# Wider spans of keys and fewer groups of queries in a banded attention, with values loaded in smaller pieces

## The reference, cut to what matters

```python
# q, k, v: (2, 8, 768, 64); n_global = 8, n_local = 96
scores = scale * np.matmul(q, k.transpose(0, 1, 3, 2))
rel = pos[:, None] - pos[None, :]
is_global = pos[None, :] < int(n_global)
is_local = (rel >= 0) & (rel < int(n_local))
keep = is_global | is_local
dist = np.where(is_global & ~is_local, float(n_local), np.abs(rel).astype(np.float32))
scores = np.where(keep, scores - slopes * dist, -1e9)
x = softmax(scores) @ v                       # then heads side by side: (2, 768, 512)

u = x + (x^T @ U @ V)^T                       # mixing over the sequence, rank 32
x = u + relu(u @ w_ch1) @ w_ch2               # 512 -> 2048 -> 512

xk = mu_k * x + (1 - mu_k) * x_prev           # x_prev: the row before
xr = mu_r * x + (1 - mu_r) * x_prev
k = relu(xk @ w_k)                            # 512 -> 1024
out = sigmoid(xr @ w_r) * (k * k @ w_v)
```

## Time and profile before

| | us |
|---|---|
| median of 3 runs | 567.49 (566.18 to 567.58) |
| the profiled execution | 570.11 |
| its span | 568.6 |
| granted clock, mean | 0.973 of 2.4 GHz |
| attention, start to about 133 us | 133 |
| matrix products after it | 435 |

### The profile page before, as it was taken

How to read it: one execution, slowest core, us unless ns; L and a number is a source line. 1 busy time by engine, 2 the same in 40 slices (tenths; PEclk the granted TensorE clock), 3 DMA queues, 4 the chain that set the end, 5 groups by cost and what they waited for, 6 DMA issues and landing times.

```text
span 568.6 us, 13272 instructions
## 1 busy us (share of the span) xinstructions
PE 527.8 (93%) x5432; PEld 490.0 (86%) x5432; DVE 192.4 (34%) x527; ACT 139.3 (24%) x408; POOL 248.7 (44%) x251
## 2 busy tenths in 40 slices
PE   2877687798999999999999999999999999999997
PEld 1655566578999999999999999999898898998996
DVE  3547654451222222222212223221253253243122
ACT  2655455551110111111111111112222221321321
POOL 2206812231720090002990056880299599599000
PEclk9879888889999999999999999999999999999999
DMA  8466444510030022000442000000000100101001
GB/s 279 168 251 251 179 178 176 215 56 3 18 131 0 0 75 74 0 0 0 148 148 74 0 1 0 0 0 0 2 1 1 55 0 18 38 1 52 3 0 55
DMA packets 14794, 37.67 MB, mean 66 GB/s; under 512 B 2080, under 2 KB 3360, under 8 KB 13728
## 3 DMA queue, kind: packets, MB, share of 16 engines
q1 hardware_dynamic: 14176, 36.24, 18.0%
q10 hardware_dynamic: 576, 0.84, 0.4%
HBM read 33.92 MB, written 3.15 MB: 65 GB/s over the span
## 4 chain that ended last, share of the span: by engine, by line
PE 92%; issue 4%; DMA 1%; DVE 1%; POOL 0%; ACT 0%; ACTq 0%; DVEq 0%; POOLq 0%
PE psum L525 24%; PE psum L537 23%; PE psum L581 12%; PE psum L590 11%; PE psum L605 6%; PE psum L381 5%; PE psum L393 3%; PE psum L419 2%; DMA k_in<-in_k 1%; PE psum L410 1%; PE psum L436 1%; PE psum L427 1%; PE psum L433 1%; PE psum L434 1%; PE psum L397 1%
## 5 line engine op out<-in xcount | busy, mean ns | idle before, releaser
L929 DVE SCALAR_TENSOR_TENSOR HL<-psum,HH 128x384 fp32r<-128x384 f32 x64 | 35.7, 558 | 176.4 <-ACT HH L724 176.4
L724 ACT ACTIVATE HH<-psum 128x384 fp32r<-128x384 f32 x64 | 31.5, 491 | 235.1 <-PE psum L525 235.1
L525 PE MATMUL psum<-UH,w1h 128*128 (+1 forms) x256 | 86.3, 337 | 1.9 <-POOL UL L1029 1.9
L537 PE MATMUL psum<-HH,w2h 128*128 128x384 f32 x256 | 86.1, 336 | 0.0
L537 PE MATMUL psum<-HL,w2h 128*128 128x384 f32 x256 | 86.1, 336 | 0.0
L525 PE MATMUL psum<-UH,w1l 128*128 (+1 forms) x256 | 86.0, 336 | 0.0
L525 PE MATMUL psum<-UL,w1h 128*128 (+1 forms) x256 | 85.9, 335 | 0.0
L537 PE MATMUL psum<-HH,w2l 128*128 128x384 f32 x256 | 85.8, 335 | 0.0
L1040 POOL TENSOR_SCALAR w1h<-raw 128x2048 fp32r<-128x2048 f32 x5 | 9.6, 1915 | 126.2 <-PE psum L537 126.2
L381 PE MATMUL psum<-k_in,q_in 64*32 64x128 f32 (+1 forms) x1536 | 30.9, 267 | 29.8 <-issue 18.6
L381 PEld LDWEIGHTS psum<-k_in,q_in 64*32 64x32 f32 x1536 | 21.0, 120 | 37.4 <-issue 25.7
(11 more groups left out here) (115 smaller groups left out, 989.5 us busy)
## 6 DMA issues: line engine op xcount, KB each, us to landing
v_in<-in_v SPq DMA_DIRECT2D x8, 1536.0 KB, 6.1
raw<-in_moe_w_ch SPq DMA_DIRECT2D x8, 1024.0 KB, 7.1
out<-result SPq DMA_DIRECT2D x12, 256.0 KB, 2.1
k_in<-in_k SPq DMA_DIRECT2D x7, 432.0 KB, 8.3
q_in<-in_q SPq DMA_DIRECT2D x7, 384.0 KB, 6.9
raw<-in_moe_w_v SPq DMA_DIRECT2D x2, 1024.0 KB, 5.2
raw<-in_moe_w_k SPq DMA_DIRECT2D x2, 1024.0 KB, 5.0
raw<-in_moe_w_r SPq DMA_DIRECT2D x1, 1024.0 KB, 5.1
```

The lines of the kernel that those rows point to most:

```text
L525: mm = pe.matmul(bank[4 + f % 2][:, 0:BLK], w[:, kt, f * P:(f + 1) * P], x[:, kt, ds(blk * BLK, BLK)], start=kt == 0 and n == 0, stop=kt = ...
L537: mm = pe.matmul(bank[d][:, 0:BLK], w[:, f, d * P:(d + 1) * P], x[:, f % 2, :], start=f == 0 and n == 0, stop=f == FQ - 1 and n == 2)
L724: act.activation(HH[:, f % 2, :], bank[4 + f % 2][:, 0:BLK], ACT.Relu).then_inc(hid_high, 1)
L929: dve.scalar_tensor_tensor(out=HL[:, f % 2, :], in0=bank[4 + f % 2][:, 0:BLK], scalar=0.0, in1=HH[:, f % 2, :].bitcast(F32), op0=ALU.max, ...
```

## The change

Groups have 64 queries instead of 32, so a tile has two. A group's span is 160 keys (BAND + GROUP). A tile's block of columns is 160 + 32 = 192, and the two tiles of a head lie side by side in 384 columns, the first with its globals behind the span, the second with them ahead. So each head's 384 columns are turned as three blocks of 128: the middle one holds the globals of both tiles and, of each, the 32 keys of the span that are beyond 128. The outer ones hold 128 keys of a tile each. The values are laid out by the host in the same way: `v_in` has two copies of 128 rows in place of four, and `v_rest` has the rows for the middle block, for every unit and group. `v_in` is loaded in two pieces, one for each group, behind `v_rest`. The copy of the globals on ScalarE is gone; both evacuations now move 384 columns. SP waits for pair 0's queries and keys before it loads values. The distances of even tiles other than the first are copied to a third block once.

```diff
-GROUP = 32
-BAND = P - GROUP
+GROUP = 64
+BAND = 96
+REST = 2 * GROUP - BAND
...
-        def turned_at(i, h):
-            return 3 * h + i
+        def main_at(i, j):
+            at = i * (2 * WIN - P) + j * GROUP
+            return slice(at, at + GROUP)
+
+        def rest_at(j):
+            return slice(P + j * GROUP, P + (j + 1) * GROUP)
+
+        def dist_of(i, t):
+            at = WIN * (0 if t == 0 else 2 - i)
+            return dist[:, at:at + WIN]
...
-                sp.dma_start(v_in[:, p % 2, :, :, :, :], vp[p]).then_inc(v_landed[p % 2], 16)
-                sp.dma_start(v_glob[:, p % 2, :, :], vg[p]).then_inc(v_landed[p % 2], 16)
+                sp.dma_start(v_rest[:, p % 2, :, :, :, :], vr[p]).then_inc(v_landed[p % 2], 16)
+                for j in range(GROUPS):
+                    sp.dma_start(v_in[:, p % 2, j, :, :, :], vm[p][:, j, :, :, :]).then_inc(v_landed[p % 2], 16)
...
             sp.dma_start(counts_i[:, :], counts.partition_broadcast(P)).then_inc(counts_in, 16)
+            sp.wait_ge(qk_in[0], 32)
             load_v(0)
             load_qk(1)
...
-                    for at, w in ((BAND, GLOB), (None, P)):
+                    for frm, w, to in ((t * P, SPAN, i * (WIN + GLOB)), (None, GLOB, SPAN + i * GLOB)):
                         for j in range(GROUPS):
                             for h in range(2):
                                 r = slice(h * D, (h + 1) * D)
-                                frm = t * P + j * GROUP if at is None else at
-                                to = i * WIN + (GLOB if at is None else 0)
+                                k_at = BAND if frm is None else frm + j * GROUP
                                 mm = pe.matmul(bank[SCORE_BANKS[h]][group(j), to:to + w],
                                                q_in[r, p % 2, t * P + j * GROUP:t * P + (j + 1) * GROUP],
-                                               k_in[r, p % 2, frm:frm + w], start=True, stop=True)
+                                               k_in[r, p % 2, k_at:k_at + w], start=True, stop=True)
                 mm.then_inc(qk_done, 1)
...
                 for h in range(2):
                     pe.wait_ge(exp_done, 2 * n + h + 1)
-                    for i in range(2):
-                        mm = pe.transpose(bank[TURN_BANKS[h]][:, i * P:(i + 1) * P],
-                                          probs[:, n % 2, i, h, GLOB:WIN], ident[:, :])
-                mm.then_inc(pt_done, 1)
-                pe.wait_ge(glob_kept, n + 1)
-                pe.transpose(bank[TURN_BANKS[0]][:, 2 * P:3 * P],
-                             probs_glob[:, n % 2, :], ident[:, :]).then_inc(pt_done, 1)
-
-            def weigh_globals(n):
-                p = n // UNITS
+                    for c in range(0, 2 * WIN, P):
+                        mm = pe.transpose(bank[TURN_BANKS[h]][:, c:c + P], probs[:, n % 2, h, c:c + P], ident[:, :])
+                    mm.then_inc(pt_done, 1)
+
+            def weigh_rest(n):
+                p, u = n // UNITS, n % UNITS
                 if n >= 1:
                     pe.wait_ge(norm_done, n)
-                if n % UNITS == 0:
-                    pe.wait_ge(v_landed[p % 2], 32 * (p // 2 + 1))
-                pe.wait_ge(ptevac[0], n + 1)
-                for j in range(GROUPS):
-                    for i in range(2):
-                        r = slice(i * 2 * GLOB, (i + 1) * 2 * GLOB)
-                        pe.matmul(WEIGHTED[group(j), i, :], probs_t[r, n % 2, 2, group(j)],
-                                  v_glob[r, p % 2, :, :].rearrange("p h d -> p (h d)"), start=True, stop=False)
+                if u == 0:
+                    pe.wait_ge(v_landed[p % 2], 48 * (p // 2 + 1))
+                for h in range(2):
+                    pe.wait_ge(ptevac[h], n + 1)
+                    for j in range(GROUPS):
+                        for i in range(2):
+                            r = slice(i * GROUP, (i + 1) * GROUP)
+                            pe.matmul(WEIGHTED[group(j), i, h * D:(h + 1) * D], probs_t[r, n % 2, h, rest_at(j)],
+                                      v_rest[r, p % 2, u, j, h, :], start=h == 0, stop=False)
 
             def weigh(n):
                 p = n // UNITS
-                pe.wait_ge(ptevac[1], n + 1)
                 for h in range(2):
                     for i, t in unit_tiles(n):
                         for j in range(GROUPS):
                             mm = pe.matmul(WEIGHTED[group(j), i, h * D:(h + 1) * D],
-                                           probs_t[:, n % 2, turned_at(i, h), group(j)],
+                                           probs_t[:, n % 2, h, main_at(i, j)],
                                            v_in[:, p % 2, j, t, h, :], start=False, stop=h == 1)
                 mm.then_inc(pv_done, 1)
...
-            def keep_globals(n):
-                act.wait_ge(exp_done, 2 * n + 2)
-                act.activation(probs_glob[:, n % 2, :].rearrange("p (a g) -> p a g", g=GLOB),
-                               probs[:, n % 2, :, :, 0:GLOB].rearrange("p i h g -> p (i h) g"),
-                               ACT.Copy).then_inc(glob_kept, 1)
-
             def evac(n):
-                act.wait_ge(pt_done, 2 * n + 1)
+                act.wait_ge(pt_done, 2 * n + 2)
                 if n >= 2:
                     act.wait_ge(pv_done, n - 1)
-                act.activation(probs_t[:, n % 2, 3:5, :].rearrange("p a n -> p (a n)"),
-                               bank[TURN_BANKS[1]][:, 0:2 * P], ACT.Copy).then_inc(ptevac[1], 1)
+                act.activation(probs_t[:, n % 2, 1, :], bank[TURN_BANKS[1]][:, 0:2 * WIN],
+                               ACT.Copy).then_inc(ptevac[1], 1)
...
+            def even_tiles():
+
+                dve.tensor_copy(dist[:, 2 * WIN:2 * WIN + SPAN], dist[:, WIN + GLOB:2 * WIN]).then_inc(dist_step, 1)
+                dve.tensor_copy(dist[:, 2 * WIN + SPAN:3 * WIN], dist[:, WIN:WIN + GLOB]).then_inc(dist_step, 1)
...
                 for h in range(2):
+                    if h == 1 and n >= 2:
+                        dve.wait_ge(pt_done, 2 * (n - 2) + 2)
                     for i, t in unit_tiles(n):
-                        m = dve.tensor_tensor_reduce(probs[:, n % 2, i, h, :],
+                        m = dve.tensor_tensor_reduce(probs[:, n % 2, h, i * WIN:(i + 1) * WIN],
                                                      bank[SCORE_BANKS[h]][:, i * WIN:(i + 1) * WIN],
-                                                     dist[:, min(t, 1), :], slopes[2 * (p % PPB) + h], 3.0e38,
+                                                     dist_of(i, t), slopes[2 * (p % PPB) + h], 3.0e38,
                                                      ALU.add, ALU.min, neg_max[:, n % 2, i, h:h + 1])
                     m.then_inc(max_done, 1)
 
             def evac(n):
-                dve.wait_ge(pt_done, 2 * n + 2)
+                dve.wait_ge(pt_done, 2 * n + 1)
                 if n >= 2:
                     dve.wait_ge(pv_done, n - 1)
-                dve.tensor_copy(probs_t[:, n % 2, 0:3, :].rearrange("p a n -> p (a n)"),
-                                bank[TURN_BANKS[0]][:, 0:3 * P]).then_inc(ptevac[0], 1)
+                dve.tensor_copy(probs_t[:, n % 2, 0, :], bank[TURN_BANKS[0]][:, 0:2 * WIN]).then_inc(ptevac[0], 1)
...
+    for t in range(tiles):
+        for j in range(P // GROUP):
+            span = ahead[:, t * P + j * GROUP:t * P + (j + 1) * GROUP + BAND]
+            rest = laid["v_rest"][:, t % 2 * GROUP:(t % 2 + 1) * GROUP, t // 2, j]
+            if t % 2:
+                main, left, at = span[:, REST:], span[:, :REST], slice(GLOB, GROUP)
+                glob = slice(0, GLOB)
+            else:
+                main, left, at = span[:, :P], span[:, P:], slice(0, REST)
+                glob = slice(REST, GROUP)
+            laid["v"][:, :, j, t] = main
+            rest[:, at] = left
+            rest[:, glob] = v[:, :, :GLOB].transpose(0, 2, 1, 3)
```

More of the change, by code:

```diff
@@ L53, in block_kernel @@
     GROUPS = P // GROUP
-    WIN = GLOB + P
+    SPAN = BAND + GROUP
+    WIN = GLOB + SPAN
     FIRST = 2 * P
@@ L151, in block_kernel @@
         region = Region(y_at)
-        reach = region("reach", [P, 2, WIN])
-        far = region("far", [P, 2, WIN])
-        grid = region("grid", [P, P])
-        place = region("place", [P, P])
-        behind = region("behind", [P, P])
+        reach = region("reach", [P, 2 * WIN])
+        far = region("far", [P, 2 * WIN])
+        grid = region("grid", [P, SPAN])
+        place = region("place", [P, SPAN])
+        behind = region("behind", [P, SPAN])
         key = region("key", [P, GLOB])
@@ L773, in reaches @@
                 dve.wait_ge(reach_step, GROUPS + 3)
-                dve.tensor_tensor(reach[:, 1, GLOB:WIN], grid[:, :], behind[:, :], ALU.max).then_inc(reach_step, 1)
+                dve.tensor_tensor(reach[:, WIN + GLOB:2 * WIN], grid[:, :], behind[:, :], ALU.max).then_inc(reach_step, 1)
                 dve.wait_ge(reach_step, GROUPS + 4)
```

(18 more changed lines are left out.)

57 lines of the change are left out of this document (32 added, 25 removed).

## The result

The changed kernel takes 539.62 us (median of 4 runs, 538.57 to 540.81), the one before on the same chip 566.86 (4 runs, 566.18 to 567.58): a ratio of 0.952, 95% interval 0.9492 to 0.9548, or 27.2 us less. The forecast was 537, with a range of 526 to 554.

A forecast was written before the change was run, and what follows sets the result against it. TensorE bounds the kernel and, in the attention, runs out of instructions. Stalls -18, clock -10, start -2.8, work 0, loads +2 give -28.8 us, another way -30.3; -30 was taken from 567.5: 537 us, range 526 to 554.

The forecast's parts named there:

- Stalls: TensorE's waits for instruction blocks in the attention: 22.3 us before, 4 left at 13 crossings, 18 us won.
- the wait of 4.9 shrinks to about 4.9/4 = 1.2 us: An instruction block waits only behind the values' load in progress, so smaller loads cut its wait from 4.9 to 1.2 us.
- The other term of the step: With fewer instructions a unit, a block of 256 on TensorE lasts 5.0 us, where it was 3.2.
- Rival A: The block still comes after everything queued; a stall of 2.3 us stays in each pair: +18, 555 us; chance 0.14.
- Clock: Without long stalls TensorE's clock stays up in the attention: of 14.2 us lost, 4 left, 10 won.
- Start: SP's wait for pair 0 brings first scores to 5.3 us and unit 3's to 15.2 from 17.99: -2.8 us.
- Work per unit: TensorE's scores, weighing, rest and transposes in an attention unit sum to 0, between -0.4 and +0.4 us.
- Later loads: Scaled queries of later pairs are covered; pairs 3 and 4, behind a chunk, come 1.8 us late each: +2 us.
- Rival B: 64-wide calls on TensorE run alone, not side by side: +2.3 us a unit, 55 us, 592 us; chance 0.04.
- rival C: TensorE's stalls follow time, not instruction count; only start and loads count: 566 us; chance 0.04.
- E: Better than said: scores go by count, no stall, clock up: -12 us, 525 us; chance 0.08.
- D: VectorE or the pair's load paces the units at 3.6 us: 7 us more, 544; chance 0.70 together with the forecast.

The follow-up runs named there:

- after_no_add_half_rows: The changed kernel without VectorE's addition of 1e-9 to the sums, and with v_in in four loads of 192 KB, not two of 384: 537.97 us, ratio 0.9472.
- before_pieces: The kernel before, with a pair's values in four loads of 384 KB in place of one of 1536 KB: 566.56 us, ratio 0.9964.
- before_fewer: The kernel before, with the narrow score calls left out after pair 0 (170 instructions a unit, not 234): 551.42 us, ratio 0.9711.
- before_fewer_pieces: The kernel before, with narrow score calls left out after pair 0 and the values in four loads of 384 KB: 552.67 us, ratio 0.9733.
- after_no_add: The changed kernel without VectorE's addition of 1e-9 to the sums ahead of the reciprocal: 537.3 us, ratio 0.9462.

## Why the prediction was right, and where it was not

**Stalls: right in size, wrong in one step of the reason.** Issue on the chain fell from 24.0 to 3.0 us, 21 where 18 were forecast. The step that failed is "the wait of 4.9 shrinks to about 4.9/4 = 1.2 us". DMA queues of the changed kernel from 62.1 to 64.9 us and from 64.9 to 66.0 us (packets, MB, share):

```profile
q1 hardware_dynamic: 388, 1.06, 99.2%
```

```profile
q1 hardware_dynamic: 145, 0.40, 98.4%
q8 instruction: 1, 0.02, 5.3%
```

TensorE entered a block at 62.1 us. For 2.9 us no packet of instructions moved, though the values came in three loads, and the next block came when they were through (so too at 75.7 and 85.5 us). The wait is about 3 us, not 1.2. That is 1.9 us less than before, and the values are fewer by 28% (1152 KB for 1600), which by itself would be 1.4 of it; TensorE also entered its block later after the values' issue (1.7 us, 0.9 before).

The size of the pieces has a share all the same. What queue 1 moved from the issue of the values to the block's packet, in the change from 60.4 to 64.95 us and in after_no_add_half_rows from 58.3 to 61.75:

```profile
q1 hardware_dynamic: 433, 1.20, 77.6%
```

```profile
q1 hardware_dynamic: 412, 0.77, 70.8%
```

The values are 1152 KB, 1.18 MB. In the change all of them had moved; with half rows 0.4 MB of them had not. In the last three pairs the block waited 1.7, 1.6 and 1.7 us there (entered at 60.05, 70.26 and 80.45 us), where the change has 2.9, 3.1 and 2.7 (62.1, 72.6 and 82.9). From the issue of the values to the packet it was 3.5 to 3.8 us with half rows, 4.6 to 5.3 in the change and 4.9 to 6.0 in the kernel before. So smaller pieces do shorten the wait, by less than in proportion, and "when the values are through" is no rule either. Loads and rows were made smaller together; which of the two counts was not tested. While the block waited, the 16 DMA engines moved about as many rows in both kernels: 388 packets of queue 1 in the change (the fence above), 370 with half rows.

The other term of the step also came out otherwise: the block in progress from 62.1 us on,

```profile
62.08:68.10 6.02, 6.02 (x143) 5.28 (x136) 4.55 (x25) 4.48 (x18) 0.35 (x1) 1.00 0.83 318
```

lasts 6.0 us and not the forecast 5.0, because two turns and most of two halves of the mixing fall in it, 20 matmuls that take 2.7 us of it; the block behind it lasts 4.5. (The row counts more than 256 records, since it takes in calls that began before it.) With the packet's 1.0 us and some 1.4 from its end to the first instruction, as in the kernel before (96.64 to 98.01 us), a wait of 2.9 makes 5.3 us, under 6.0. With the old 4.9 it would be 7.3, so by this estimate both terms were needed. From outside, the number weighs more than the pieces: before_pieces gave 0.4%, before_fewer 2.9%, before_fewer_pieces 2.7%.

How a block's place behind other packets is decided was not measured by itself and stays open. Rival A's "after everything queued" is contradicted: queries and keys were still moving when the block came. The Trainium skill, DMA: Bandwidth & Descriptors, Queues, rings and completion order, has each DMA engine change queues after a packet of typically 9 to 17 descriptors. The traces agree in so far as smaller rows let the block in earlier; if a row is one descriptor, which no trace shows, the 23 or 24 rows that each engine moved before it (388 and 370 over 16) are more than that.

**Clock: right.** One stretch at 0.50 is left ahead of the hidden layer, in the changed kernel:

```profile
17.42:20.84 3.42, 3.42 (x50) 2.83 (x46) 3.01 (x12) 2.27 (x9) 2.14 (x2) 0.50 0.90 323
```

3.4 us of busy work at half clock cost 1.7, against 14.2: 12.5 won, 10 forecast.

**Start: over-estimated.** First scores at 5.08 us (5.3 forecast), but those of unit 3 at 16.48, not 15.2: 1.5 us won at that point, not 2.8, and nothing that can be measured in the end. The forecast's own terms, 7.2 and 6.0 and 0.9, make 14.1 and not 15.2, so this step was wrong by 2.4 us; the keys of pair 1 landed at 15.4 us (7.51 plus 7.93), not at 13.2.

**Work per unit: inside its bounds, a little high.** A unit is up to 0.3 us longer than before (3.38 for 3.08), where zero was taken. Turns took 0.81 us (0.87 forecast; 0.70 before). Weighing took 0.61, against 0.58 before, but against 0.45 in the units with the sums of the mixing. Scores took 0.91, not 0.75, where they took 0.88: half the calls and 20% more area came to nearly the same. The rest's calls took 0.26 on the chain and some 0.4 to 0.46 with what they overlap, against 0.22. I had also written that the maxima keep their 160 columns; they have 192, and ScalarE's exponential went from 417 to 444 ns. Both engines stay hidden outside pairs 3 and 4.

**Later loads: right in kind.** The keys of pair 3 took 9.35 us behind a chunk and its scaled queries came at 37.73 us, for which TensorE waited 0.6 us. The addition blocked by GpSimd (1.6, 2.4, 0.9 and 2.4 us in four units) was missed altogether; it was there before as well (3.35 us at most, of which 1.8 lie on the chain of before at 45.21), beside stalls that cost more.

**The sum.** 21 + 12.5 + 1.5 is 35.0 and the attention is 31.2 shorter, so 3.8 went to longer units, late queries and the addition; these three were not separated. Forecast was 30, and the median fell by 27.2: the other 4 are the two profiled runs, 3.3 us above and 0.7 below their medians. That the forecast came out within 3 us owes something to luck, since stalls and clock gave 5.5 us more than forecast and start, units and the addition took them back. Rival A's stall of over 2 us in each pair did not come. Rival B is excluded (16 weighing records in 0.61 us, 38 ns apart, where its sign was over 60), rival C by before_fewer, E by the sum. D came in part: in pairs 3 and 4 VectorE set the pace, through the blocked addition.

## What to carry to other kernels

Where an engine stalls with no semaphore behind it, count its instructions between stalls: if they come to the same number each time, it is starved of instructions, and the first remedy is that this many must last longer than their fetch, by larger calls. Cutting the data loads up shortened the wait for a block here as well, but 384 KB pieces by themselves bought 0.4%. Shorten a stage and look at the chain again for what it hid; here it was an instruction on four columns, blocked by GpSimd, and removing it was worth 2.3 us in one comparison and 4.7 (with half rows) in another. Put a wait at the start only if what it delays isn't needed next.

## What the runs showed of the hardware that was not expected

In these kernels small float32 calls with 64-column weights cost by the load and not by the keys that they cover: the same scores took 0.91 us in 32 loads and 2.46 in 80, 32 ns for each load more. At 32-column weights, 64 loads took 0.88 to 0.93 us and 32 took 0.60 to 0.68 (with a fifth of the area gone as well). In three of these four cases the time is 0.43 to 0.48 ns for each weight column loaded (2048, 2048, 5120); the fourth, 1024 columns, takes 0.59 to 0.66, so that this isn't the whole rule.

A VectorE tensor_scalar on four columns waited up to 2.47 us (3.35 before) for GpSimd; the reciprocal did not in any of its 24 executions in after_no_add.

256 instructions of TensorE took 2.8 to 3.2 us in the kernel before, and their successor was late by up to 1.4 us in quiet queues and by 2.4 to 3.5 behind 1.5 MB of values. From the issue of a pair's values to that packet it took 4.9 to 6.0 us with 1600 KB in rows of mostly 12 KB, 4.6 to 5.3 with 1152 KB in 3 KB rows, and 3.5 to 3.8 when two thirds of these came in 1.5 KB rows (last three pairs of each).
